# Attention feeding a two-layer network on one core: another layout of the first batch, sums of the last 64 keys by matmuls

## The reference

```python
scores = cap * tanh(q @ k.T / 8 / cap)              # (4, 12, 448, 448)
attn = exp(scores - max(scores))                    # over keys
attn = attn / (sum(attn) + 1e-9)
x = (attn @ v), heads side by side                  # (1792, 768)
h = x @ w_in                                        # (768, 2048)
r = maximum(h, 0)
y = (s * r * r + b) @ w_out                         # (2048, 768), all float32
```

## Time and profile before

| | us |
|---|---|
| median of 3 runs (lowest, highest) | 653.55 (652.8, 655.07) |
| profiled execution | 654.5 |
| its span | 652.7 |
| TensorE busy | 632.1 (97%) |
| VectorE busy | 345.3 (53%) |
| ScalarE busy | 246.1 (38%) |
| GpSimd busy | 37.0 (6%) |

### The profile page before, as it was taken

One profiled execution on the slowest core, in us unless ns is written; L12 is line 12 of the kernel. 1 busy time (PEld: TensorE's weight loads), 2 busy tenths in 40 slices (PEclk: granted clock), 3 DMA queues, 4 the chain that ended last, 5 costly groups with the idle time before them and its releaser, 6 DMA issues.

```text
span 652.7 us, 7957 instructions
## 1 busy us (share of the span) xinstructions
PE 632.1 (97%) x3146; PEld 490.6 (75%) x3146; DVE 345.3 (53%) x587; ACT 246.1 (38%) x255; POOL 37.0 (6%) x28
## 2 busy tenths in 40 slices
PE   5989989979999999999999999999999999999998
PEld 3333657656767676767677999999999999999997
DVE  1699999997767667767665433222432131213111
ACT  4788444544444544454541322222321121213110
POOL 0122333420000000000000000000000000000000
PEclk8899989998999999999999999999999999999999
DMA  5344143422222222313111411213152233215002
GB/s 167 116 140 140 57 141 115 158 62 99 87 69 88 82 73 83 100 57 101 40 57 44 159 49 49 68 54 109 50 191 57 57 121 105 57 30 183 1 1 84
DMA packets 32148, 57.14 MB, mean 88 GB/s; under 512 B 3952, under 2 KB 23920, under 8 KB 32112
## 3 DMA queue, kind: packets, MB, share of 16 engines
q1 hardware_dynamic: 31680, 56.64, 26.8%
q10 hardware_dynamic: 432, 0.00, 0.0%
HBM read 40.11 MB, written 16.52 MB: 87 GB/s over the span
## 4 chain that ended last, share of the span: by engine, by line
PE 81%; DVE 13%; ACT 3%; issue 2%; DMA 1%; POOLq 0%; POOL 0%; ACTq 0%; DVEq 0%
PE hid L345 10%; PE hid L347 10%; PE hid L346 10%; PE scores L360 8%; PE scores L361 8%; PE scores L359 8%; PE pv L304 5%; PE scores L270 5%; PE pv L360 4%; PE pv L361 4%; PE pv L359 4%; PE scores L289 2%; DVE w_hi L503 2%; DVE e_sum L522 1%; PE pv L316 1%
## 5 line engine op out<-in xcount | busy, mean ns | idle before, releaser
L345 PE MATMUL hid<-x_hi,w_hi 128*128 128x448 f32 x384 | 144.6, 377 | 6.5 <-POOL w_lo L669 6.5
L347 PE MATMUL hid<-x_hi,w_lo 128*128 128x448 f32 x384 | 142.3, 371 | 0.0
L346 PE MATMUL hid<-x_lo,w_hi 128*128 128x448 f32 x384 | 142.2, 370 | 0.0
L360 PE MATMUL scores<-x_lo,w_hi 128*128 128x448 f32 x256 | 93.5, 365 | 0.0
L359 PE MATMUL scores<-x_hi,w_hi 128*128 128x448 f32 x256 | 93.5, 365 | 0.0
L361 PE MATMUL scores<-x_hi,w_lo 128*128 128x448 f32 x256 | 93.5, 365 | 0.0
L345 PEld LDWEIGHTS hid<-x_hi,w_hi 128*128 128x128 f32 x384 | 73.4, 191 | 24.9 <-issue 19.0
L595 DVE SCALAR_TENSOR_TENSOR x_lo<-e,const,x_hi 128x448 fp32r<-128x448 f32 x48 | 32.1, 683 | 103.8 <-ACT x_hi L447 103.8
L347 PEld LDWEIGHTS hid<-x_hi,w_lo 128*128 128x128 f32 x384 | 73.3, 191 | 6.4
L346 PEld LDWEIGHTS hid<-x_lo,w_hi 128*128 128x128 f32 x384 | 73.5, 191 | 6.0
L433 ACT ACTIVATE e<-e,const 128x1792 f32<-128x1792 f32 (+1 forms) x48 | 77.0, 1604 | 1.6
(11 more groups left out here) (67 smaller groups left out, 666.0 us busy)
## 6 DMA issues: line engine op xcount, KB each, us to landing
qk<-q_k SPq DMA_DIRECT2D x24, 448.0 KB, 3.8
hidden_scratch<-hidden_sb SPq DMA_DIRECT2D x48, 224.0 KB, 1.9
e<-hidden_scratch SPq DMA_DIRECT2D x48, 224.0 KB, 2.6
work<-w_in SPq DMA_DIRECT2D x24, 256.0 KB, 3.5
e<-w_out SPq DMA_DIRECT2D x16, 384.0 KB, 3.0
y_t<-qk SPq DMA_DIRECT2D x24, 224.0 KB, 2.0
v_sb<-v SPq DMA_DIRECT2D x24, 192.0 KB, 2.6
v_tail<-v SPq DMA_DIRECT2D x12, 64.0 KB, 2.3
```

Of the source, the lines that this page charges most:

```text
L345: nc.tensor.matmul(out, w_hi[:, j, w], x_hi[:, batch % 2, c, :], start=c == 0, stop=False)
L346: nc.tensor.matmul(out, w_hi[:, j, w], x_lo[:, batch % 2, c, :], start=False, stop=False)
L347: last = nc.tensor.matmul(out, w_lo[:, j, w], x_hi[:, batch % 2, c, :], start=False, stop=c == CT - 1)
L360: nc.tensor.matmul(y_acc(c), w_hi[:, j, w], ring(x_lo, n), start=False, stop=False)
```

## The change

It changes these things:

- PSUM is one tensor of eight banks: scores 0 to 3, hid 4 and 5, pv 6 and 7. In the first batch the last key tile's scores go to hid (pair 0: hid, and the rests to pv), the rests of later quads to banks 2 and 3, values to pv[p % 2] and the sums to the other pv bank.
- In the first batch last_scores(p+1) stands before values(p), and tail_values is done per pair instead of per two.
- The first batch's sums take the last 64 keys by two more matmuls per pair on fourths of the array; VectorE's third addition is gone there.
- Twelve chunks (tiles j = 0 and 1, EARLY) are done between pair 5 and slot 6; the slots of batch 1 then bring 14 chunks each instead of 16.
- GpSimd does the cast of w_in as well as the subtraction, ten pieces during the first batch (four of them with only the cast until the sixth pair is scaled).
- cap, s and b come in one DMA; pair 0's q and k come in two halves on two queues; the exponential behind the guard moves behind pair 0.
- Later batches: transpose and reduction of e_sum are one instruction.
- The order of SyncE's loads is rewritten.

```diff
@@ sync
-            load_qk(0)
+            sp.dma_start(qk[0:D, 0]..., q_k[0, 0, 0:D]).then_inc(qk_in[0], 16)
             load_qk(1)
             load_v(0)
             load_w_in(0)
             load_w_in(1)
+            load_qk(2)
+            load_w_in(2)
+            load_w_in(3)
             load_v(1)
-            load_qk(2)
-            for p in range(PAIRS):
+            load_v(2)
+            load_w_in(4)
+            load_qk(3)
+            load_w_in(5)
+            load_w_in(6)
+            load_v(3)
+            load_w_in(7)
+            load_w_in(8)
+            load_w_in(9)
+            for p in range(2, PAIRS):
+                load_qk(p + 2)
                 load_v(p + 2)
-                load_qk(p + 3)
-                load_w_in(p + 2)
...
@@ tensor
+            def first_scores(p):
+                pe.wait_ge(qk_in[p % QK_SLOTS], qk_loads(p))
+                reach(pe, first_read, p)
+                if p <= PAIRS:
+                    for head in range(2):
+                        row_scores(p, head, 0, head)
+                    if p % 2 and p > 1:
+                        pe.wait_ge(last_read, last_group(p - 1))
+                    for head in range(2):
+                        last = row_scores(p, head, 1, 2 + head)
...
             def sums(p):
-                out = first_banks(p)
-                pe.wait_ge(e_sum_done, 3 * (p + 1))
-                reach(pe, sums_read, p - 1)
+                out = sums_out(p)
+                pe.wait_ge(e_sum_done, adds(p))
+                reach(pe, x_done, p)
                 for head in range(2):
                     rows = slice(head * D, (head + 1) * D)
-                    last = nc.tensor.matmul(out[rows, 1, 0:S], ones[:], e_sum[:, p % 2, head, :], start=True, stop=True)
+                    nc.tensor.matmul(out[rows], ones[:], e_sum[:, p % 2, head, :], start=True, stop=False)
+                keys = slice(p % 2 * D, (p % 2 + 1) * D)
+                for head in range(2):
+                    rows = slice(head * D, (head + 1) * D)
+                    last = nc.tensor.matmul(out[rows], ones[keys], e[keys, G1 + head, :], start=False, stop=True)
                 last.then_inc(sums_done, 1)
...
             first_scores(0)
-            last_scores(0)
+            last_scores(0, G1)
+            tail_scores(0, G1 + 2)
             for p in range(PAIRS):
                 first_scores(p + 1)
+                if p + 1 < PAIRS:
+                    pe.wait_ge(last_read, last_group(p))
+                    last_scores(p + 1, G1)
                 values(p)
-                if p % 2:
-                    tail_values(p // 2)
-                last_scores(p + 1)
                 sums(p)
+                tail_values(p, 1)
+                if p % 2 and p + 1 < PAIRS:
+                    pe.wait_ge(first_read, p + 2)
+                    tail_scores((p + 1) // 2, 2)
+            for c in range(CT - 1):
+                hidden_chunk(0, c)
+            pe.wait_ge(first_read, PAIRS + 1)
+            tail_scores(PAIRS // 2, 0)
+            last_scores(PAIRS, 2)
+            for c in range(CT - 1):
+                hidden_chunk(0, CT + c)
+            for j in range(2):
+                hidden_chunk(0, CT * j + CT - 1)
...
@@ vector
-                nc.vector.transpose(turned..., e_sum[:, p % 2]...).then_inc(turned_done, 1)
-                dve.wait_ge(turned_done, m + 1)
-                nc.vector.tensor_reduce(parts[:], turned[:]..., AX.X, ALU.add)
+                nc.vector.tensor_reduce(parts[:], e_sum[:, p % 2]..., AX.X, ALU.add, apply_transpose=True)
...
             add_first_e(0)
-            add_last_e(0)
             for p in range(PAIRS):
-                w_in_high(p)
+                add_last_e(p)
+                if p == 0:
+                    dve.wait_ge(guard_done, 2)
+                else:
+                    scale_pair(p - 1)
                 add_first_e(p + 1)
-                if p % 2:
-                    scale_pair(p - 1)
                 invert_first(p)
-                if p % 2:
-                    scale_pair(p)
-                add_last_e(p + 1)
...
@@ gpsimd
+            for piece in range(CT):
+                high(piece)
+                low(piece)
+            for piece in range(CT, CT + 4):
+                high(piece)
+            pool.wait_ge(x_done, PAIRS)
+            for piece in range(CT, CT + 4):
+                low(piece)
+            for piece in range(CT + 4, PIECES):
+                high(piece)
+                low(piece)
```

More of the change, by code:

```diff
@@ L261, in _, with qk_loads, row_scores @@
         def _(pe):
-            def first_scores(p):
[L263 to L267, removed]
+            def qk_loads(p):
+                return 16 * (p // QK_SLOTS + 1 + (p % QK_SLOTS == 0))
+            def row_scores(p, head, t, bank):
+                rows = slice(head * D, (head + 1) * D)
+                i = p % QK_SLOTS
+                return nc.tensor.matmul(banks[:, bank, 0:S], qk[rows, i, 1, t * P:(t + 1) * P], qk[rows, i, 0, :],
+                                        start=True, stop=True)
@@ new lines, in first_scores @@
+            def first_scores(p):
+                pe.wait_ge(qk_in[p % QK_SLOTS], qk_loads(p))
[8 more added lines that the diff above has]
+                else:
+                    pe.wait_ge(last_read, last_group(p - 1))
+                    for t in range(FULL - 1):
+                        for head in range(2):
+                            last = row_scores(p, head, t, 2 * t + head)
+                last.then_inc(first_done, 1)
@@ L268, in first_scores, with last_scores, tail_scores @@
+            def last_scores(p, bank):
+                for head in range(2):
+                    last = row_scores(p, head, FULL - 1, bank + head)
+                last.then_inc(last_done, 1)
+            def tail_scores(quad, bank):
+                pe.wait_ge(qk_in[(2 * quad + 1) % QK_SLOTS], qk_loads(2 * quad + 1))
+                for odd in range(2):
+                    of = (2 * quad + odd) % QK_SLOTS
+                    out_rows = slice(odd * D, (odd + 1) * D)
                     for head in range(2):
@@ L269, in first_scores @@
                         rows = slice(head * D, (head + 1) * D)
[L270 to L291, removed]
@@ L293, in values @@
+                        last = nc.tensor.matmul(banks[out_rows, bank + head, 0:S], qk[rows, of, 1, FULL * P:],
+                                                qk[rows, of, 0, :], start=True, stop=True)
+                last.then_inc(tails_done, 1)
             def values(p):
@@ L303, in values, with tail_values @@
                         tile = (head * FULL + t) * D
-                        last = nc.tensor.matmul(out[rows], v_sb[:, i, tile:tile + D], e[:, tile_of(p, 2 * t + head), :],
+                        last = nc.tensor.matmul(out[rows], v_sb[:, i, tile:tile + D], e[:, tile_of(p, t, head), :],
                                                 start=t == 0, stop=False)
                 last.then_inc(main_done, 1)
[L308 to L313, removed]
+            def tail_values(first, pairs):
+                i = first // 2 % 2
+                pe.wait_ge(v_tail_in[i], 16 * (first // 4 + 1))
+                for p in range(first, first + pairs):
+                    keys = slice(p % 2 * D, (p % 2 + 1) * D)
@@ L386, in _ @@
                 if p % 2:
-                    tail_values(p // 2)
+                    tail_values(p - 1, 2)
                 if p + 1 < ALL:
-                    last_scores(p + 1)
-                for chunk in range(SHARE * c, SHARE * (c + 1)):
+                    pe.wait_ge(first_read, p + 2)
+                    if p % 2:
+                        tail_scores((p + 1) // 2, 0)
+                        last_scores(p + 1, 2)
+                    else:
+                        last_scores(p + 1, 0)
+                for chunk in range(*chunks_of(batch - 1, c)):
                     hidden_chunk(batch - 1, chunk)
@@ L499, in _ @@
         def _(dve):
[L500 to L505, removed]
             def add_first_e(p):
-                first = tile_of(p, 0)
+                first = tile_of(p, 0, 0)
                 dve.wait_ge(exp_done, 2 * p + 1)
@@ L639, in _ @@
                     add_last_e(p + 1)
-                for j in tiles_in(SHARE * c, SHARE * c + 8):
+                start, end = chunks_of(batch - 1, c)
+                for j in tiles_in(start, start + 8):
                     square((batch - 1) * JT + j)
@@ L643, in _ @@
                     invert(p + 1)
-                for j in tiles_in(SHARE * c + 8, SHARE * (c + 1)):
+                for j in tiles_in(start + 8, end):
                     square((batch - 1) * JT + j)
```

195 lines of the change are left out of this document (124 added, 71 removed).

## The result

The changed kernel takes 660.86 us (median of 4 runs, 659.96 to 662.01), the kernel before 654.27 beside it (652.8 to 655.07): ratio 1.0113, 95% interval 1.0084 to 1.0142. My forecast was 640.6 with a range of 637.5 to 647, and it gave slower a chance of 0.03. Its profiled execution has a span of 657.9 us, 5.2 more than before.

What follows compares the result with a forecast made beforehand. TensorE, busy 632.1 of 652.7 us, was taken as the bound. 11.5 us from waits in the slots and 1.5 by slot 6 put slot 12 12.9 us earlier: 640.6 from the median 653.55, range 637.5 to 647.

Steps and rivals of the forecast that it cites:

- part 1: Slots from 6 on: moving w_in's casts to GpSimd and its loads ends TensorE's waits for GpSimd, 11.5 us gained.
- odd 15.4; three of each 87.7: Slots 6 to 11 with 14 chunks: odd ones 15.4 us, even ones 13.8, three of each 87.7 together.
- the rest unchanged: From slot 12 on, forecast at 157.2 instead of 170.13 us, nothing changes in time.
- B: Rival: GpSimd's slow cast stops SyncE's queue and delays pair 4's q and k; slower than before, e.g. 656.5 us; chance 0.03.
- D: Rival: in the slots one stall for GpSimd stays, with its stretch at the lower clock; 646 us; chance 0.10.
- the waits for GpSimd: Chunks waited twice for w_in's low part, 6.5 us; with lower clock 11.5 us in two slots, forecast to go.
- The two groups on fourths: First batch, per pair: the new matmuls on fourths run beside each other, 0.85 us; the rests' values 0.80.
- A: Rival: in the first batch the fourths run one after the other, 1.6 instead of 0.8 us; 649.6 us; chance 0.07.
- C: Rival: VectorE's additions take 2.17 instead of 1.09 us beside GpSimd, about four on the path; 644.6 us; chance 0.12.
- Slot 6: Starts at 69.5 us with twelve chunks done, against 63.67 with none: 1.5 us gained.
- The first Tanh: At the start: one DMA for the constants lets it begin at 7.4 us instead of 9.30.
- The stretch at the lower clock: At the start, after TensorE's idle 10.9 to 13.1 us: one such stretch costing 1.5 us (ends 0 and 3.3).

Runs made afterwards that it cites:

- e1: The changed kernel with the load of q and k issued one turn earlier from slot 6 on (pair p+3 in turn p): 642.77 us, ratio 0.984.
- e2: The kernel before with only the load of q and k moved one turn later from slot 6 on: 661.33 us, ratio 1.0137.
- e9: The changed kernel with the load of q and k for pair p+3 put in front of turn p's last hidden store: 642.8 us, ratio 0.9824.
- e7: e3 with cap, s and b loaded by one DMA instead of three: 641.53 us, ratio 0.9803.
- e8: e7 with the first six pieces of w_in cast by VectorE, GpSimd casting from piece 6 on: 639.31 us, ratio 0.9773.
- e3: The kernel before with only the casts of w_in moved from VectorE to GpSimd: 643.93 us, ratio 0.9851.
- e6: e1 without the twelve early chunks, so slots 6 to 11 have 16 chunks again: 645.77 us, ratio 0.9866.
- e4: e1 with the guard's two ScalarE instructions back in front of the loop, before pair 0: 642.12 us, ratio 0.9829.

## Why the prediction was wrong

**The step that failed** is in part 1, "the casts go to GpSimd, the loads move". I followed the loads of w_in through SyncE's queue, each with what it waits behind, and did not do the same for the loads of q and k, which the diff moves in the same loop, from pair p+3 to pair p+2 of a turn. So the sentence "odd 15.4; three of each 87.7" had no term for them, and "the rest unchanged" was wrong too: the same load costs 1.9 us in slots behind slot 12. Odd slots need q and k two pairs ahead, because the rests of two pairs are scored together (in the kernel before the wait stands at the head of L285's group). The change left the load of pair p+2 to turn p, behind the last store of turn p-1. What was needed to see it was at hand: a load lands 3.8 us after its issue, the rests' scores come 1.7 + 2.4 + 0.8 = 4.9 us after a slot's start, and the last square of a slot can come behind an inversion, which ends several microseconds into the next slot (in the kernel before at 108.22, 6.9 us behind a slot's start). Part 1 even named the store that did it and had it "near 85", and it came at 89.65. With the store at 85 the load would have landed at about 89.2 (an estimate: 85, 0.4 from the store's issue to the load's, 3.8 to landing), just in time; the 4.65 us by which the store was later match the 4.57 us of the wait. e1, e2 and e9 show this from three sides. No rival of mine named it; B had the right queue and the wrong cause, a slow cast in front of load_qk(4). D had a stall left over in the slots, from GpSimd.

**What held**, read from the changed kernel: the waits for GpSimd went. Even slots took 13.8. The cast on GpSimd took 0.61 us undisturbed, against my 1.3, so the spare time was larger still. The two groups on fourths took about the price of halves, from start to start 0.80 for the new one (L396) and 0.85 for the rests' values (L381); the forecast had 0.85 and 0.80:

```profile
L776 POOL CAST w_hi<-work x24: 603/614/1476, 8.7 to 135.0; 128x512 fp32r<-128x512 f32 x24
```

```profile
36.38 0.97 PE L396 MATMUL banks<-e,ones 64*64 64x448 f32 x4
...
37.18 0.92 PE L381 MATMUL banks<-e,v_tail 64*64 64x448 f32 x4
...
38.03 2.53 PE L315 MATMUL banks<-qk 64*128 64x448 f32 x12
```

A period of the first batch took 16.52 us (31.52 to 48.04), 16.6 forecast, with TensorE 94% busy. A falls by the 0.80. C falls too: the four additions before 26 us took 1.32, 1.88, 1.52 and 1.33 instead of 1.09, 1.7 us more in all and not 4, and TensorE waited 0.3 us for one of them. Slot 6 began at 70.62, 69.5 forecast, and that it is so near is in part luck, since two errors have opposite signs. The first Tanh came at 9.55 instead of 7.4: 1.3 us are the table load behind the scores' wait, which I had overlooked, and 0.8 the first scores, which began at 6.38 and not at 5.55. The stretch at the lower clock at 14 us, for which I had 1.5, did not come. In e1 slot 12 starts at 158.34 against my 157.2, and e1's 642.77 lies 2.2 above my 640.6: the other terms came out right in sum, and the one left out was worth 18.1 us.

The Trainium skill's page "GPSIMD Engine Reference" (section 4.1) puts one-input operations on GpSimd near line rate; the cast's 0.61 us for 512 elements is less than half of the subtraction's 1.27, though VectorE's cast of the same size took 0.42, so the trace agrees in kind. What it says on contention with VectorE's instructions that have two SBUF inputs (section 1) is borne out by e7 and e8: 1.60 against 1.07 us for L520, 1.14 against 1.43 for L513, each time the longer one where GpSimd works beside it.

**What the parts are worth**, as far as shown: the casts on GpSimd in the slots 11.1 us (e3), one DMA for the constants 2.4 with the better clock that came with it and about 1.2 without (e7 against e3), early chunks 3.0 within the new layout (e6). The new layout with fourths as a whole brought nothing against the old first batch (e7 is 0.4% ahead of e1 by ratio, with overlapping intervals; 0.65 us of that may be the guard's place, e4). Its banks alone weren't tried.

## What to carry to other kernels

When a diff reorders a queue of DMA issues, list for every load in it, also the ones that look merely tidied, the first instruction that reads it and the issue that stands in front of it; a load behind a store inherits the store's wait for computation. A pipeline that works two items together needs its loads one item earlier than its loop suggests. And ask of each moved cast or addition which engine sets the pace in that stage: the same cast won 11.1 us on GpSimd in one stage and lost about 2 us there in another. Where two engines slow each other, it counts which instruction the slow one is: the addition that the next engine waits for, or one with idle time in front of it.

## What the runs showed of the hardware

A reduction with transpose in one instruction takes no longer than the plain reduction of the same tile (1.10 us; before, 1.10 for the transpose and 1.09 for the reduction, so one takes the time of half the pair):

```profile
L651 DVE TRANSPOSE_TENSOR_REDUCE parts<-e_sum x18: 1094/1100/1111, 73.5 to 346.0; 128x28 f32<-128x896 f32 x18
```

Pauses of TensorE of 1.6 and 1.75 us at 10 and 13 us left the clock at 1.00 in the changed kernel, and pauses no longer than these, 0.3 and 1.75 us, were followed by the lower level in e4 (mean 0.66 from 13 to 18 us). So whether such a pause costs clock could not be told from its length here; why is left open.
